# The last product of a fused kernel by seven half-block products in place of eight, in quarter tiles of 256 tokens

## The reference

```python
scores = scale * q @ k.T                      # 4 batches, 8 heads, 576 tokens, 64 features
x = (scores * Dmat) @ v                       # Dmat: gamma**(i-j) for i >= j, else 0
x = x as (2304 tokens, 512 features)
# first layer, d_ff 1536
xn = x / sqrt(mean(x*x) + 1e-6) * rms_g
x = (silu(xn @ w_gate) * (xn @ w_val)) @ w_out
# second layer, d_ff 2048
h = x @ w_in
g = where(h >= 1, h, where(h <= -1, 0, (h + 1)**2 / 4))
out = g @ w_out                               # (2304, 2048) @ (2048, 512)
```

## Time and profile before

| | |
|---|---|
| median of 3 runs (lowest to highest) | 914.8 us (911.91 to 916.41) |
| the profiled execution, its own time | 914.95 us |
| its span, first to last instruction | 913.2 us |
| granted TensorE clock, mean | 0.994 of full speed |
| busy time: PE, PEld | 884.4 us, 837.0 us |
| busy time: DVE, ACT, POOL | 471.2 us, 435.7 us, 261.3 us |
| first matmul of `chain_o` to its last | 713.8 us to 909.9 us |

### The profile page before, as it was taken

The page is one execution under the profiler, slowest core; times in us unless marked ns, Lnnn a source line. Parts: engine busy times, 40 slices in busy tenths (PEclk is TensorE's granted clock), DMA queues, the critical chain, the costliest instruction groups (busy, mean ns, idle before and its releaser), DMA issues.

```text
span 913.2 us, 16544 instructions
## 1 busy us (share of the span) xinstructions
PE 884.4 (97%) x6944; PEld 837.0 (92%) x6944; DVE 471.2 (52%) x606; ACT 435.7 (48%) x688; POOL 261.3 (29%) x179
## 2 busy tenths in 40 slices
PE   6898999999999999999999988999999999999998
PEld 5787999999999999999999988999999888888886
DVE  3497865477954653622243487765657632222220
ACT  2555654445654555512132257877779732222220
POOL 0235764445864664000041321422224200000000
PEclk9998999999999999999999999999999999999999
DMA  9985133333336336334624134242449654444440
GB/s 247 237 240 146 47 99 99 99 98 98 100 98 235 100 98 210 128 105 149 214 74 138 45 136 145 105 150 104 151 161 293 198 155 116 116 115 116 116 125 25
DMA packets 121179, 124.00 MB, mean 136 GB/s; under 512 B 5425, under 2 KB 91569, under 8 KB 121105
## 3 DMA queue, kind: packets, MB, share of 16 engines
q1 hardware_dynamic: 121104, 122.94, 43.2%
HBM read 80.45 MB, written 42.47 MB: 135 GB/s over the span
## 4 chain that ended last, share of the span: by engine, by line
PE 82%; DVE 5%; DMA 5%; ACT 3%; issue 2%; POOL 1%; SPq 1%; ACTq 0%; DVEq 0%
PE pair L614 13%; PE pair L616 13%; PE pair L615 13%; PE pair L746 7%; PE pair L747 7%; PE pair L748 7%; PE pair L712 6%; PE pair L713 6%; PE pair L714 6%; DMA a_kt<-ktok 2%; PE pair L528 1%; DVE cb L1320 1%; PE pair L558 1%; PE pair L564 1%; PE pair L543 1%
## 5 line engine op out<-in xcount | busy, mean ns | idle before, releaser
L614 PE MATMUL pair<-xc,wc 128*128 128x288 f32 x672 | 199.4, 297 | 0.5 <-ACT cp L870 0.2
L615 PE MATMUL pair<-xc,wc 128*128 128x288 f32 x672 | 198.2, 295 | 0.0
L616 PE MATMUL pair<-xc,wc 128*128 128x288 f32 x672 | 197.6, 294 | 0.0
L870 ACT ACTIVATE cp<-pair 128x576 f32<-128x576 f32 x160 | 103.4, 647 | 152.9 <-PE pair L616 147.1
L1408 POOL TENSOR_TENSOR wc<-wt,wc 128x512 fp32r<-128x512 f32 x84 | 122.9, 1486 | 91.9 <-ACT wc L803 77.7
L614 PE MATMUL pair<-xc,wr 128*128 128x288 f32 x448 | 133.9, 299 | 6.9 <-ACT cp L870 6.3
L615 PE MATMUL pair<-xc,wr 128*128 128x288 f32 x448 | 132.2, 295 | 0.0
L616 PE MATMUL pair<-xc,wr 128*128 128x288 f32 x448 | 131.7, 294 | 0.0
L614 PEld LDWEIGHTS pair<-xc,wc 128*128 128x128 f32 x672 | 125.9, 187 | 1.4 <-issue 1.3
L616 PEld LDWEIGHTS pair<-xc,wc 128*128 128x128 f32 x672 | 126.6, 188 | 0.0
L615 PEld LDWEIGHTS pair<-xc,wc 128*128 128x128 f32 x672 | 126.1, 188 | 0.0
(11 more groups left out here) (94 smaller groups left out, 1451.2 us busy)
## 6 DMA issues: line engine op xcount, KB each, us to landing
b_scratch<-cb SPq DMA_DIRECT2D x32, 576.0 KB, 2.9
bv_r<-b_scratch SPq DMA_DIRECT2D x18, 1024.0 KB, 5.8
a_scratch<-cb SPq DMA_DIRECT2D x24, 576.0 KB, 2.9
av_r<-a_scratch SPq DMA_DIRECT2D x8, 1728.0 KB, 8.3
wt<-wB SPq DMA_DIRECT2D x72, 128.0 KB, 2.9
a_k<-kT SPq DMA_DIRECT2D x16, 288.0 KB, 7.9
a_q<-qT SPq DMA_DIRECT2D x16, 288.0 KB, 7.0
a_v<-vtok SPq DMA_DIRECT2D x16, 288.0 KB, 7.8
```

What stands on the lines that cost most here:

```text
L614: pe.matmul(o, wh, xh, start=FIRST[i] and j == 0, stop=False, skip_group_check=True)
L615: pe.matmul(o, wh, xl, start=False, stop=False, skip_group_check=True)
L616: mm = pe.matmul(o, wl, xh, start=False, stop=j == 1, skip_group_check=True)
L870: act.activation(copied(g, n)[:, :, :], pair[(X, Q, X, X)[n]][:, :, 0:HALF], ACT.Copy).then_inc(s_c, 1)
```

## The change

The output product is made by seven half-block products as well. The weights (2048 by 512) are cut into blocks A11, A12, A21, A22 of 256 output columns, and each block's eight pieces into four groups r of two pieces (`NGRP`). A tile T is 256 tokens, two halves of 128; there are nine (`NTO`). A quarter (T, r) is tile T with group r: seven products of 2 pieces by 3 matmuls, 42 matmuls with 256 columns. There are 36 quarters; tiles 0 and 1 take turns (quarters 0 to 7), the later tiles go one after the other. The sums of the four quarters of a tile gather in PSUM, in four banks.

```diff
+QUARTERS = [(T, r) for r in range(NGRP) for T in range(2)] + [(T, r) for T in range(2, NTO) for r in range(NGRP)]
+ORDER = (0, 3, 5, 1, 4, 2, 6)
+W_ORDER = (A11, A12, A22, S1, S3, S2, S4)
+def bq_of(k):
+    return (1, 2, 0, 3)[(k - 1) % 4] if k else 0
...
 # SP
-            def load_wq(f, n):
-                src = wC.rearrange("(f k) p c -> p f k c", k=2)[:, f:f + n, 1, :]
-                sp.dma_start(wq_raw[f][:, 0:n, 1, :], src).then_inc(d_wq[f], 16)
+            def load_wq(r):
+                w = wC.rearrange("(f k) p c -> p f k c", k=2)[:, :, 1, :]
+                for dst, kk, n in ((w_last(r, A11), 0, 0), (wa21[r][:, :, :], 0, 1),
+                                   (w_last(r, A12), 1, 0), (w_last(r, A22), 1, 1)):
+                    f = FC // 2 * kk + 2 * r
+                    sp.dma_start(dst, w[:, f:f + 2, n * WIDE:(n + 1) * WIDE]).then_inc(d_wq[r], 16)
...
-                sp.dma_start(bv_raw[i][:, 1, :, :], b_s[:, :, k * P:(k + 1) * P]).then_inc(d_bl[i], 16)
+                for at, kk, th in ((LOW[B11], 0, 0), (LOW_B12, 0, 1), (LOW[B22], 1, 1), (LOW[B21], 1, 0)):
+                    f = FC // 2 * kk + 2 * r
+                    t = (2 * T + th) * P
+                    sp.dma_start(bt[i][:, at, :, :], b_s[:, f:f + 2, t:t + P]).then_inc(d_bl[i], 16)
...
+                if n == GC - 2:
+                    load_b(0)
+                if n >= GC - 3:
                     sp.wait_ge(s_p, 7 * g)
...
+                    load_wq(n - (GC - 3))
                 if n:
                     store_b(g - 1, 0)
...
                     store_b(g - 1, 1)
+            sp.wait_ge(s_p, 7 * (GALL - 1) + 5)
+            load_b(1)
             sp.wait_ge(s_p, 7 * GALL)
+            sp.wait_ge(s_wS, 4)
+            load_wq(3)
+            sp.wait_ge(s_d, 4 * GALL)
+            sp.wait_ge(d_as[0], stored(GALL - 2))
             load_b(2)
+            store_b(GALL - 1, 0)
+            sp.wait_ge(s_o, 7)
+            load_b(3)
+            store_b(GALL - 1, 1)
+            sp.wait_ge(d_as[1], stored(GALL - 1))
+            load_b(4)
...
+            for k in range(1, NQ):
+                if k + 4 < NQ:
+                    sp.wait_ge(s_o, 7 * (k + 1))
+                    load_b(k + 4)
+                if k == last_quarter(T):
+                    store_out(T, 1)
+                    store_out(T, 0)
+                    T += 1
 # PE
+            def quarter(k):
+                T, r = QUARTERS[k]
...
+                for n, i in enumerate(ORDER):
...
+                    for c in range(2):
+                        xh, xl = bh[b][:, HIGH[i], c, :], bl[b][:, LOW[i], c, :]
...
+                        pe.matmul(o, xh, w[:, i, 0, c, :], start=first and n % 2 == 0, stop=False,
+                                  skip_group_check=True)
+                        pe.matmul(o, xh, w[:, i, 1, c, :], start=False, stop=False, skip_group_check=True)
+                        mm = pe.matmul(o, xl, w[:, i, 0, c, :], start=False, stop=last, skip_group_check=True)
 # ACT, after the last step's copies
+            parabola(GALL - 1, 0)
+            b_hi(1, False)
+            b_hi(1, True)
+            parabola(GALL - 1, 1)
+            wq_hi(1, (6,))
+            parabola(GALL - 1, 2)
+            b_hi(2, False)
+            b_hi(2, True)
+            parabola(GALL - 1, 3)
+            b_hi(3, False)
+            b_hi(3, True)
+            wq_hi(2, range(7))
...
 # DVE
+            def b_sums(k):
+                dve.tensor_tensor(t1_t3, b12_b22, b11_b12, ALU.subtract).then_inc(s_bT, 1)
+                dve.wait_ge(s_bT, 3 * k + 1)
+                dve.tensor_tensor(t[:, LOW[T2], :], t[:, LOW[B22], :], t[:, LOW[T1], :], ALU.subtract).then_inc(s_bT, 1)
+                dve.wait_ge(s_bT, 3 * k + 2)
+                dve.tensor_tensor(t[:, LOW[T4], :], t[:, LOW[T2], :], t[:, LOW[B21], :], ALU.subtract).then_inc(s_bT, 1)
...
+                if n >= GC - 3:
+                    wq_sum(n - (GC - 3), S1)
+                    wq_sum(n - (GC - 3), S3)
                 if n == GC - 2:
-                    wq_lo(5)
+                    b_sums(0)
                 c12(g)
...
+                if n >= GC - 3:
+                    wq_sum(n - (GC - 3), S2)
+                    wq_sum(n - (GC - 3), S4)
...
+            b_sums(1)
+            joined(GALL - 1, 0)
+            b_lo(1)
+            joined(GALL - 1, 1)
+            b_sums(2)
+            joined(GALL - 1, 2)
+            b_lo(2)
+            joined(GALL - 1, 3)
+            b_sums(3)
+            b_lo(3)
+            wq_lo(2)
...
 # POOL
+            wq_lo(0)
+            b_lo(0)
+            wq_lo(1)
+            for k in range(1, 4):
+                b_lo(k)
+            wq_lo(2)
+            for k in range(4, 6):
+                b_lo(k)
+            wq_lo(3)
+            for k in range(6, NQ):
+                b_lo(k)
```

More of the change, by code:

```diff
@@ L51 @@
 B_BY_POOL = (B11, B21, B22)
-WQ_BY_DVE = (5, 8, 11, 13, 15)
-WQ_BY_POOL = tuple(f for f in range(FC) if f not in WQ_BY_DVE)
+WIDE, NGRP = DM // 2, 4
+NTO = NTOK // (2 * P)
+QUARTERS = [(T, r) for r in range(NGRP) for T in range(2)] + [(T, r) for T in range(2, NTO) for r in range(NGRP)]
+NQ = len(QUARTERS)
+ORDER = (0, 3, 5, 1, 4, 2, 6)
+W_ORDER = (A11, A12, A22, S1, S3, S2, S4)
+LOW = {B11: 0, T1: 3, B22: 2, T3: 5, B21: 4, T4: 6, T2: 7}
+LOW_B12 = 1
+HIGH = {T1: 0, T3: 1, T2: 2, B11: 3, B22: 4, B21: 5, T4: 6}
 NORM_AT = (3, 5)
@@ L87, in slot_of, with uses, last_quarter @@
     return (7 * (un - 2 * UB) + i) % RING
+def bq_of(k):
+    return (1, 2, 0, 3)[(k - 1) % 4] if k else 0
+def uses(k):
+    return sum(bq_of(n) == bq_of(k) for n in range(k + 1))
+def last_quarter(T):
+    return QUARTERS.index((T, NGRP - 1))
 def build(nc, qT, kT, ktok, vtok, qdec, mask, kdec, cdec, rmsg, wB, wC, out):
@@ L217, in build @@
         d_wo = {f: sem(f"d_wo{f}") for f in wo_raw}
-        d_wq = {f: sem(f"d_wq{f}") for f in wq_raw}
+        d_wq = [sem(f"d_wq{r}") for r in range(NGRP)]
         d_as = [sem(f"d_as{i}") for i in range(2)]
@@ L222, in build @@
         d_yl = [sem(f"d_yl{i}") for i in range(2)]
-        d_bl = [sem(f"d_bl{i}") for i in range(3)]
+        d_bl = [sem(f"d_bl{i}") for i in range(4)]
         d_out = [sem(f"d_out{i}") for i in range(2)]
@@ L498, in _ @@
+            sp.wait_ge(d_as[0], stored(GALL - 2))
             load_b(2)
[L500 to L505, removed]
-            for k in range(NBLK):
-                if k + 3 < NBLK:
-                    sp.wait_ge(s_o, k + 1)
-                    load_b(k + 3)
-                store_out(k)
+            store_b(GALL - 1, 0)
@@ L512, in _ @@
             for i in range(2):
-                sp.wait_ge(d_out[i], 16 * NBLK // 2)
+                sp.wait_ge(d_out[i], 32 * len(range(i, NTO, 2)))
         @block.tensor
@@ L755, in _ @@
+            for k in range(NQ):
+                quarter(k)
         @block.scalar
@@ L943, in _ @@
                 if 2 * UB + 5 <= g < 2 * UB + 11:
[L944 removed]
+                    wo_hi(2 * (g - 2 * UB - 5))
                 if g == GB - 1:
@@ L1395, in _ @@
+            T = 0
+            for k in range(4, NQ):
+                if T < NTO and k == last_quarter(T) + 3:
+                    gather(T)
+                    T += 1
+                b_sums(k)
+                b_lo(k)
+                if k == 4:
+                    for i in (S1, S3, S2, S4):
+                        wq_sum(3, i)
+                if k == 5:
+                    wq_lo(3)
+            for T in range(T, NTO):
+                gather(T)
         @block.gpsimd
@@ L1472, in _ @@
                 unit(un)
-            for f in WQ_BY_POOL:
-                wo_lo(f, 1)
+            wq_lo(0)
+            b_lo(0)
+            wq_lo(1)
[4 more added lines that the diff above has]
+                b_lo(k)
+            wq_lo(3)
+            for k in range(6, NQ):
+                b_lo(k)
 def _decay_tables():
```

320 lines of the change are left out of this document (181 added, 139 removed).

## The result

The changed kernel took **939.16 us** (median of 4 runs, 938.97 to 942.45), where the kernel before took 913.79 beside it (4 runs, 911.91 to 916.41): ratio 1.0284, 95% interval 1.0248 to 1.0320, **slower by 25.4 us**. The prediction was 914.5 with a range of 907 to 922: it is wrong, and no rival that was slower came near. The profiled execution has a span of 937.0 us, 23.8 more than before.

A forecast was written before the change was run, and what follows sets the result against it. PE, busy 97% of the span, was taken as the bound. Terms -14.5 + 2.2 + 8.9 + 0.5 + 2.9 - 0.2 = -0.2 (lists: 0.4 earlier) against 914.95 profiled gave 914.6, in effect 914.5 us; range 907 to 922.

The forecast's parts named there:

- The distance of 120 ns: PE, output product: starts of 256-column matmuls lie 120.0 ns apart, 106.7 for the columns and 13.3 fixed.
- the 14.5 us saved: PE, output product: 1512 matmuls of 256 columns take 181.4 us where 864 of 512 took 195.9.
- The wait before quarter 1 for POOL's low parts: After quarter 0, PE waits until POOL finishes `b_lo(1)` at 729.9: 8.9 us lost.
- DVE's sums in front of `c12`: Steps 14 and 15: S1, S3 and `b_sums(0)` delay `c12`; PE gets its result at 705.3, wanted at 704.4.
- Rival (b): Step 14: weight group lands late, holding DVE before `c12`, then ACT and SP; 918.0 to 922.9 us, chance 22%.
- The price of an issue on SP: SP, new transfers: 0.64 us to issue each, with 0.47 kept as the low end.
- signs named for being wrong: New profile: waits at every tile, quarter 1 starting before 726 or after 734, or a distance other than 120 ns.
- Prices of the rest: Durations taken from rows for DVE, ACT, POOL, SP and transfers; `b_sums` on DVE 1.6 us, POOL's 1024 elements 2.5.
- What lies hidden: From quarter 8: every engine fits into 5.04 us a quarter, DVE needing 3.2, POOL 2.5 (3.3 at worst).
- Should that cover go, each us over it is lost eight times: From quarter 8, after a `gather`: about 3 us of cover are left; any excess over it costs eightfold.
- `load_b(1)` stands on SP behind `store_b(14, 1)`: Before quarter 1: the token load waits for step 14's last join and store, landing at 720.9; part of 8.9 us lost.
- the clock's loss: Quarter 1, after PE's pause: 3.4 us lost at half clock, taken up by waits before quarters 5 and 6.

The follow-up runs named there:

- e7_tok1_w_sp: Changed kernel, token low parts from quarter 1 and those of weight groups 2, 3 on DVE; loads of quarter 1 and weight group 1 moved ahead on SP: 920.72 us.
- e10_after_late: Changed kernel with only the SP order of `e7_tok1_w_sp` and weight group 2's four sums behind quarter 2's low parts on DVE: 939.07 us.
- e8_no_wlow: Changed kernel without the weights' low parts (their matmuls take the high parts), all token low parts on DVE, POOL idle in this stage: 915.11 us.
- e9_late_sums: `e7_tok1_w_sp` with the four sums of weight group 2 moved from step 15 to behind quarter 2's low parts on DVE: 919.18 us.
- e3_tok8_dummy: Changed kernel with DVE making all token low parts from quarter 8, plus 28 unused POOL subtractions of 1024 elements: 956.95 us.
- e5_tok8_set: Changed kernel with DVE making all token low parts from quarter 8, plus 28 unused POOL memsets of 1024 elements: 931.99 us.

## Why the prediction was wrong

**Right.** The distance of 120 ns and the 14.5 us saved. The wait before quarter 1 for POOL's low parts, 8.9 forecast and 10.9 measured, and shorter ones before quarters 5 (0.5 and 0.6) and 6. The clock at 0.50 in quarter 1. DVE's sums in front of `c12` do hold PE up, though by 2.36 us where 0.9 was forecast: one of the two took 1.78 us and the other 1.09, for 0.68. Rival (b), a late weight group, didn't happen: DVE's wait for it ended at 700.55, where 701.7 was forecast, about as much earlier as this execution was ahead of the one before (1.2 us). The price of an issue on SP was too high, without effect here: the four of a token load took 1.9 us in the median, where 2.6 were forecast. Two of the signs named for being wrong came true: waits recur at every tile, and quarter 1 starts after 734.

**The step that failed** is in "Prices of the rest": "`b_sums` is 0.69 + 0.49 + 0.43 = 1.6 us", the 3.2 us for DVE under "What lies hidden", and every other DVE price of that kind, taken as if POOL's work beside it didn't matter. Measured in the steady part, `b_sums` takes 3.6 us (0.68 + 2.51 + 0.43) in three quarters of four, and with it one round of DVE's list takes 5.01 of the 5.04 us; the round with a `gather` takes 5.98, and so a tile takes 21.02 us in place of 20.16. "Should that cover go, each us over it is lost eight times" had the place right; the cover was priced wrong. In steps 13 to 15 and quarters 0 to 7, 22 low parts of weights and 8 of tokens lie on POOL beside sums, joins and combinations on DVE. Taking POOL's low parts away one kind after the other took off 4.6, 8.5 and 3.5 us behind quarter 0, half of the 33.9; the 5.9 us of steps 13 to 15 fell to 2.9 only where no low part of a weight was made. The overlap that the prediction counted on, POOL's low parts beside DVE's work at no cost to DVE, is what failed.

The rows could have told it. In the earlier trace rows the DVE subtraction of 1024 elements has a maximum of 2207 ns over a median of 1220 (it starts at 703.78, while a POOL subtraction runs from 703.16 to 704.90), and POOL's weights 1680 in the median over 1285. I read the second as POOL being slower "when DVE works beside it", put 3.3 us for it as the worst case, and asked neither what the DVE instruction of 2207 had waited for nor whether it goes both ways. The 3.3 was too much (at most 2.83 was seen); the hold fell on DVE, whose time nobody had put in doubt.

**A second step was only half of the cause:** "`load_b(1)` stands on SP behind `store_b(14, 1)`", given for quarter 1's wait. In the changed kernel the forecast chain is in the trace: DVE waits 0.91 us for this transfer, then come the sums, the high parts and POOL. But DVE's own list, held by POOL, ends less than a us before it. `e7_tok1_w_sp` loads 4.8 us sooner and quarter 1 waits as long, and `e10_after_late`, with the transfer early, ends where the changed kernel does. Only in `e8_no_wlow`, without the hold, does the transfer alone come last, by 3.11 us. **A third,** smaller: the clock's loss wasn't absorbed. Quarters 1, 4 and 6 are 2.5, 1.6 and 2.4 us longer than 5.04 (a wait of 0.6 before quarter 5 not counted), and 1.6 were lost in step 15: 8.0 in all, because there were four pauses, of 2.4, 10.9, 4.7 and 6.7 us, and not one.

**What stays open.** In `e9_late_sums` 17.2 us are still lost behind quarter 0, and 5.7 before it. In the wait of 3.6 before quarter 1 DVE is still held (its three sums take 4.1 us for 1.5); but 11.0 of the 17.2 are lost from quarter 2 on, where POOL is idle. The windows of `e7_tok1_w_sp` show DVE full with its own work, among it 14 low parts of weights, 16 sums and all the tokens' parts; that its amount sets the waits is borne out by the two reorderings, which gave back what they won, but I didn't measure it by taking such work away alone. I didn't find a split of the work that frees it, and none of these versions beats the kernel before. `e8_no_wlow` takes away the hold and the weights' low parts together, so of its last 6.6 us (17.2 less 10.6) it isn't told apart what each is worth. Its whole loss, 2.9 + 10.6 = 13.5, is near the 14.5 that the prediction had from its lists with the same prices, but it lies in part elsewhere (1.6 us before quarter 5 and 1.7 before quarter 10, 2.0 of clock in quarter 1), so it bears out the unheld prices only roughly.

## What to carry to other kernels

Two elementwise engines are not always two resources: here a subtraction moved to POOL was paid by DVE too, wherever DVE's instruction beside it had both inputs in SBUF. Before giving POOL such a part, add its time to DVE's need for those instructions and ask if DVE has that slack; where it hasn't, as here, DVE alone was quicker: 1024 elements take it 1.2 us, and POOL's took 2.4 and held DVE for as much as 2.1. A row whose median or maximum is far above its minimum may be a wait in disguise: look for what ran beside it. And where an engine is full, reordering its list moved the wait and didn't remove it, in both kernels tried.

## What the runs showed of the hardware

- A DVE subtraction with both inputs in SBUF stands still while a POOL subtraction runs: 256 elements took up to 2.51 us for 0.42, 512 took 2.38 for 0.68 (`e3_tok8_dummy`), and POOL's own 1024 took 2.83 for 2.39 where DVE was first. DVE instructions with one input in PSUM (0.42 beside a POOL instruction of 2.41) aren't held, and a POOL memset (0.955) and a DVE subtraction (1.23, both inputs in SBUF) run beside each other with neither longer (`e5_tok8_set`).
- An instruction whose result nobody uses cost 25 us in 28 quarters, and nothing (ratio 1.0006) in a kernel where DVE has room.
- Matmuls of fp32r with a weight load each have 13.3 ns beside their columns at 256 as at 288 and 512 columns: 120 ns, 133.3 ns and 226.7 ns.
- After a pause of PE of 2.36 us the granted clock was 0.55 for the next 3.8 us, and the matmuls of 288 columns started 240 ns apart in place of 133.3: 1.6 us lost on top of the 2.36.
